# Turning the probabilities in 32x32 blocks on VectorE, and summing the values by matmuls of 32 rows, in the attention stage of a fused attention and expert kernel

## The chip, the cores and the metric

The kernel runs on one core of one Trainium2 chip. The time of a run is the device time of one execution in microseconds (us). Five engines work side by side and meet at semaphores: TensorE (PE; its weight loads are shown apart as PEld), VectorE (DVE), ScalarE (ACT), GpSimd (POOL) and SyncE (SP), which issues most DMAs.

## The reference

Three stages follow one another, and their only output is that of the last:

```python
scores = q @ k.T / sqrt(64) + bias[h]        # 4 batches x 8 heads, 576 positions, 64 dims
attn = exp(scores - max) / sum               # softmax over the 576 keys
x = attn @ v                                 # -> 2304 tokens of 512
x = one expert of 8 for each token (relu MLP of 1024, weighted by its gate)
out = gated FFN of width 1536 on the RMS-normed x
```

The bias of a head comes from a small MLP of 32 hidden units on log(1+|i-j|)/log(1+i). All inputs and outputs are float32. The change touches only `attn @ v`.

## The kernel before, in words

The attention stage works on pairs: 16 pairs of heads, one pair (two heads of one batch) after the other. `each_pair` (L417) writes out pairs 0, 1, 14 and 15 and runs pairs 2 to 13 in a loop of two pairs. A pair has five slots: in slots 0 to 3 (s in the code) 128 queries of head 0 and 128 of head 1, and in slot 4 (`MIX`) the last 64 queries of both heads as one tile. A tile of 128 queries of one head is a unit, so a pair has 9 units (`TPP`).

A unit goes through these steps:

- `scores` (L434, PE): four matmuls of 288 columns (eight in the mixed unit) into PSUM banks 0 to 3. q and k are split into a high and a low part in the type fp32r, and each operand is taken in one pass.
- `add_bias` (L605, DVE): one custom instruction that adds the bias, writes `a_sc` and takes the row's minimum (of the negated scores).
- `exps` (L668, ACT): the exponentials into `a_pr`, with the row sum beside them. `a_pr` holds two slots.
- `turn` (L538, PE): nine transposes of 128x128 a slot, three each into PSUM banks 4, 5 and 6. After them the keys lie on the partitions.
- `keep` (L680, ACT, banks 4 and 6) and `keep_middle` (L615, DVE, bank 5): copies from PSUM into `a_pt`, which holds all 576 x 576 turned probabilities of two heads, for two pairs.

Once a pair, in the next pair's slots:

- `values` (L549, PE): for 256 queries in slot 1 and 320 in slot 3, ten fp32 matmuls each: 128 rows of keys, 64 columns of weights (v), the two heads in the left and right half of the array. The trace shows each as two matmul records. They sum in PSUM bank 7.
- `keep_out` (L692, ACT): copies of the sums into `a_ot`.
- `turn_back` (L567, PE): five matmuls that turn 128 tokens back and also give the router's logits.
- `normal` (L630, DVE): the reciprocals of the sums and two multiplications into `a_xp`, which SP stores as tokens.

Nothing but the order in which each engine's function is written, and the semaphores, sets the order of the work. On every engine the work for the next unit stands in front of the work on this slot: in slot s PE first does `scores` of slot s+1. The semaphores named in the prediction: `a_b` counts units whose bias is added, `a_e` units whose exponentials are done, `a_x` halves of `normal`, `a_oe` copies of `keep_out`.

GpSimd splits q and k of a later pair (`split_k` L361, `split_q` L379) out of what SP has loaded (`load_qk` L314); SP's order in a pair is load_qk for the pair after next, the stores of the pair before in two parts, and between them v of the next pair (`load_v` L321). Each fourth pair SP also reloads the bias of two heads.

## Time and profile before

| | us |
|---|---|
| median of 3 runs | 1076.95 |
| lowest, highest | 1076.26, 1078.61 |
| the profiled execution's own time | 1076.09 |
| its span, first to last instruction | 1074.2 |
| TensorE's mean granted clock | 0.994 of 2.4 GHz |
| bias stage, until about | 60 us |
| first transposes of pair 0, last of pair 15 | 63.2 and 329.2 us |
| expert and FFN stages | from 339 us |

PE is busy for 97% of the span, DVE for 69%, ACT for 44%, POOL for 19%. PE's busy time counts a matmul from its start to its modelled end, and matmuls overlap, so it says that PE has work in hand and not how fast that goes. A record's mean duration is longer than the distance at which records follow one another; where the prediction speaks of the distance, it divides a stretch by its records.

### The profile page before, as it was taken

What the parts mean: (1) busy time and instruction counts of PE and PEld (TensorE: products, weight loads), DVE (VectorE), ACT (ScalarE), POOL (GpSimd) and SP (SyncE); (2) the same over time, 40 slices, a digit from 0 to 9 for tenths busy, and PEclk for the clock granted to TensorE, in tenths of its full rate; (3) what the DMA queues carried; (4) which work ended last, traced back from release to release, by engine and by line L of the source; (5) the groups of instructions that cost most, each with busy time, mean ns of one, the idle gap of its engine ahead of it and who ended that gap; (6) DMA issues with size and microseconds to landing.
All of it is one profiled execution on the core that took longest, in us unless ns stands there. A gap on an engine that the chain in (4) does not pass through costs nothing.

```text
span 1074.2 us, 23115 instructions
## 1 busy us (share of the span) xinstructions
PE 1045.0 (97%) x7161; PEld 937.6 (87%) x7162; DVE 740.3 (69%) x1252; ACT 476.7 (44%) x975; POOL 203.6 (19%) x197
## 2 busy tenths in 40 slices
PE   5989999999999899999999999999999999999997
PEld 1368888888887899999999999999999999999996
DVE  8975656656564747757464499887777777767765
ACT  7987777777772525645343343131211211121111
POOL 2036444535330411222121000001000100100101
PEclk9999999999999899999999999999999999999999
DMA  4983755656411844534322160002100100100000
GB/s 144 303 231 87 188 120 116 187 114 187 110 44 42 304 160 166 199 102 145 114 90 81 56 231 1 1 0 81 39 20 0 59 0 4 55 0 0 30 1 30
DMA packets 84455, 103.14 MB, mean 96 GB/s; under 512 B 46817, under 2 KB 58129, under 8 KB 84417
## 3 DMA queue, kind: packets, MB, share of 16 engines
q1 hardware_dynamic: 80384, 89.30, 28.3%
q0 software_dynamic: 4032, 13.37, 3.6%
q8 instruction: 19, 0.31, 0.1%
q14 instruction: 20, 0.16, 0.0%
HBM read 77.26 MB, written 25.40 MB: 96 GB/s over the span
## 4 chain that ended last, share of the span: by engine, by line
PE 89%; DVE 2%; issue 1%; POOL 1%; ACT 1%; DMA 0%; POOLq 0%; DVEq 0%; ACTq 0%
PE psum L1733 27%; PE psum L1741 13%; PE psum L1246 11%; PE psum L1255 10%; PE psum L563 8%; PE psum L446 8%; PE psum L546 7%; PE psum L576 2%; PE psum L1232 1%; DVE f_eg L1688 0%; PE psum L1294 0%; DMA e_xin<-x_tokens,e_col 0%; PE psum L876 0%; DVE r_inq L991 0%; POOL e_xin L1198 0%
## 5 line engine op out<-in xcount | busy, mean ns | idle before, releaser
L1688 DVE RECIPROCAL f_eg<-f_eg 128x384 f32<-128x384 f32 x72 | 183.4, 2547 | 0.0
L1656 ACT ACTIVATE f_eg<-psum 128x384 f32<-128x384 f32 x72 | 35.4, 492 | 312.0 <-PE psum L1733 312.0
L611 DVE CUSTOM_DVE_ANT_0 a_sc<-psum,a_bias 128x576 f32<-128x576 f32 x144 | 105.4, 756 | 65.6 <-PE psum L446 59.4
L1733 PE MATMUL psum<-f_x,f_ghi 128*128 (+1 forms) x576 | 147.5, 337 | 0.4 <-DVE f_x L1549 0.4
L1733 PE MATMUL psum<-f_x,f_vhi 128*128 (+1 forms) x576 | 146.1, 334 | 0.0
L674 ACT ACTIVATE a_pr<-a_sc,a_nmax 128x576 f32<-128x576 f32 x144 | 111.1, 772 | 26.5 <-DVE a_nmax L611 21.8
L1733 PEld LDWEIGHTS psum<-f_x,f_ghi 128*128 128x128 f32 x576 | 105.8, 188 | 6.6 <-DVE f_x L1549 0.6
L1625 POOL DMA_INDIRECT out<-f_ob,f_cols x18 | 18.2, 1009 | 464.9 <-ACT f_ob L1642 316.9
L1733 PEld LDWEIGHTS psum<-f_x,f_vhi 128*128 128x128 f32 x576 | 104.0, 188 | 0.0
L446 PE MATMUL psum<-a_khi,a_qs 128*128 128x288 f32 x320 | 96.4, 322 | 0.8 <-issue 0.3
L1733 PE MATMUL psum<-f_x,f_glo 128*128 (+1 forms) x288 | 97.1, 337 | 0.0
L1733 PE MATMUL psum<-f_x,f_vlo 128*128 (+1 forms) x288 | 96.2, 334 | 0.0
L546 PE MATMUL psum<-ident,a_pr 128*128 128x128 f32 x720 | 93.0, 273 | 0.7 <-ACT a_pt L690 0.5
L1347 ACT ACTIVATE e_hhi<-psum 128x288 fp32r<-128x288 f32 x72 | 29.7, 412 | 135.3 <-PE psum L1246 134.2
L446 PE MATMUL psum<-a_klo,a_qs 128*128 128x288 f32 x320 | 87.9, 295 | 0.0
L1684 DVE TENSOR_SCALAR f_eg<-f_eg 128x384 f32<-128x384 f32 x72 | 26.4, 367 | 88.6 <-ACT f_eg L1656 87.4
L1255 PE MATMUL psum<-e_hhi,e_w2hi 128*128 128x288 f32 x288 | 87.4, 303 | 0.0
L1246 PE MATMUL psum<-e_xhi,e_w1hi 128*128 128x288 f32 x288 | 87.3, 303 | 0.0
L563 PE MATMUL psum<-a_pt,a_v 128*64 128x256 f32 (+1 forms) x640 | 84.7, 411 | 1.3 <-DVE a_xp L643 0.8
L1741 PE MATMUL psum<-f_ohi,f_alo 128*128 128x512 f32 x216 | 85.4, 396 | 0.0
L1246 PE MATMUL psum<-e_xlo,e_w1hi 128*128 128x288 f32 x288 | 85.4, 297 | 0.0
L1741 PE MATMUL psum<-f_olo,f_ahi 128*128 128x512 f32 x216 | 85.3, 395 | 0.0
(245 smaller groups left out, 2354.4 us busy)
## 6 DMA issues: line engine op xcount, KB each, us to landing
e_raw<-ew SPq DMA_DIRECT2D x16, 1024.0 KB, 5.5
bias_ihj<-b_res SPq DMA_DIRECT2D x36, 288.0 KB, 2.7
a_qraw<-q SPq DMA_DIRECT2D x32, 288.0 KB, 5.1
a_kraw<-k SPq DMA_DIRECT2D x32, 288.0 KB, 5.7
a_bias<-bias_ihj SPq DMA_DIRECT2D x16, 576.0 KB, 7.0
xn_t<-e_yn SPq DMA_DIRECT2D x8, 576.0 KB, 3.1
a_v<-v SPq DMA_DIRECT2D x32, 128.0 KB, 2.4
x_tokens<-a_xp SPq DMA_DIRECT2D x64, 64.0 KB, 1.7
```

The source lines that it names most:

```text
L446: mm = e.matmul(s_ps[:, h, half, 0:HALF], qs[:, u, c:c + P], k[:, u, a * S + half * HALF:a * S + (half + 1) * HALF], start=(i == 0), stop= ...
L546: mm = e.transpose(t_ps[g][:, P * k:P * k + P], pr[:, w, c:c + P], ident[:, :])
L563: mm = e.matmul(o_ps[64 * h:64 * h + 64, 0:n], vv[:, u, k, 64 * h:64 * h + 64], pt[:, u, block, q:q + n], start=(k == 0), stop=(k == 4))
L611: e.tensor_tensor_reduce(sc[:, h, :].rearrange("p (a s) -> p a s", a=2), s_ps[:, h, :, 0:HALF], bias[:, 2 * s + h, :].rearrange("p (c s) - ...
L674: mm = e.activation(pr[:, w, S * h:S * h + S], sc[:, h, :], ACT.Exp, bias=nmax[:, h:h + 1], scale=-1.0, accum_out=sums[:, u, 2 * s + h:2 * ...
L1246: mm = e.matmul(bank[:, 0:BT], w[:, k, :], x[:, u, k, :], start=(k == 0 and n == 0), stop=(k == KD - 1 and n == 2))
L1255: mm = e.matmul(banks.y[:, k, 0:BT], w[:, k * P:(k + 1) * P], h[:, f % 3, :], start=(f == 0 and n == 0), stop=(f == KF - 1 and n == 2))
L1347: e.activation(self.hhi[:, f % 3, :], self.banks.h[f % 2][:, 0:BT], ACT.Relu).then_inc(self.s_hh, 1)
L1656: e.activation(self.eg[:, k % 2, :], self.g_ps[k % 2][:, 0:CHUNK], ACT.Exp, scale=-1.0).then_inc(self.s_e, 1)
L1688: e.reciprocal(x, x).then_inc(self.s_c, 1)
L1733: mm = e.matmul(acc[:, 0:CHUNK], a, b, start=(q == 0 and i == 0), stop=(q == KD - 1 and i == 2))
L1741: mm = e.matmul(self.o_ps[t], x, y, start=(f == 0 and i == 0), stop=(f == KFF - 1 and i == 2))
```

## The change

`turn` moves to DVE. One instruction (`transpose`, for each unit) turns 18 blocks of 32x32 within each group of 32 partitions, from `a_pr` in SBUF to `a_pt` in SBUF; there are 9 a pair. PE's 45 transposes a pair and the copies `keep` and `keep_middle` are gone, and so is the extra ACT instruction of the mixed slot. Since a block stays in its group of 32 partitions, group g of `a_pt` holds, for all 18 blocks of 32 keys, only the queries 32g to 32g+31 of each tile.

`values` therefore takes 32 rows at a time. For each of 18 blocks of keys, 4 groups and 2 heads there is one fp32 matmul of 32 rows, 64 columns of weights and 128 or 160 moving columns: 144 a pair, each summed over 18 blocks in the bank (4 to 7) of its group. They are dealt out over slots 1, 2 and 3, six blocks (48 matmuls) a visit. `keep_out`, `turn_back` and both halves of `normal` come once a pair, at slot 4. `turn_back` now writes to banks 4 and 5.

v must lie in all four groups of partitions, so `load_v` copies a pair's v four times (a host-side reordering makes each copy contiguous). v of pair 0 is loaded at the start of the attention stage and no longer during the bias stage.

On PE, around slot 1, where the sums of the pair before begin. a_pt is the turned probabilities, a_pr the probabilities, a_khi and a_klo the two parts of k; this is the order before:

```order
L563 MATMUL psum<-a_pt,a_v 64x256 [waits a_x]
L563 MATMUL psum<-a_pt,a_v 64x256 x9
L441 REGISTER_ALU
L446 MATMUL psum<-a_khi,a_qs 128x288 [waits a_b]
L446 MATMUL psum<-a_klo,a_qs 128x288
L446 MATMUL psum<-a_khi,a_qs 128x288
L446 MATMUL psum<-a_klo,a_qs 128x288
L542 REGISTER_ALU [waits a_e]
L546 MATMUL psum<-ident,a_pr 128x128 [waits a_t0]
L546 MATMUL psum<-ident,a_pr 128x128 x2
```

and this the beginning of the same place after the change, on PE:

```order
L438 MATMUL psum<-a_khi,a_qs 128x288
L438 MATMUL psum<-a_klo,a_qs 128x288
L534 ISA
L535 ISA [waits a_v1]
L538 ISA [waits a_t]
L547 MATMUL psum<-a_pt,a_v 64x160 [waits a_x]
L547 MATMUL psum<-a_pt,a_v 64x128
L547 MATMUL psum<-a_pt,a_v 64x160
L547 MATMUL psum<-a_pt,a_v 64x128 x2
```

The matmuls of 64x256 have become 48 of 64x160 and 64x128, between the same two groups of score matmuls, and the transposes behind them have left PE.

On DVE, from the bias of slot 4 (a_bias4) to the next pair's slot 0 (a_bias0), before the change:

```order
L611 ISA a_sc,a_nmax<-psum,a_bias 128x576 [waits a_bias4]
L611 ISA a_nmax 128x1
L635 ISA
L636 RECIPROCAL a_rinv<-a_sums 128x9 [waits a_e]
L637 RECIPROCAL a_rinv<-a_sums 128x1
L638 ISA
L640 REGISTER_ALU [waits a_r]
L641 ISA [waits a_bk]
L642 REGISTER_ALU [waits a_st01]
L643 TENSOR_TENSOR a_xp<-psum,a_rinv 128x288 [waits a_pa]
L618 ISA
L627 COPY a_pt<-psum 128x3x128 [waits a_o,a_t]
```

and after it, on DVE, from the second bias of the next pair's slot 0 to the end of the pair:

```order
L589 ISA a_sc,a_nmax<-psum,a_bias 128x576 [waits a_e,a_bias0]
L589 ISA a_nmax 128x1
L601 STREAM_TRANSPOSE a_pt<-a_pr 128x18x32 [waits a_e]
L609 ISA
L610 RECIPROCAL a_rinv<-a_sums 128x9 [waits a_e]
L611 RECIPROCAL a_rinv<-a_sums 128x1
L612 ISA
L614 REGISTER_ALU [waits a_r]
L615 ISA [waits a_bk]
L616 REGISTER_ALU [waits a_st01]
L617 TENSOR_TENSOR a_xp<-psum,a_rinv 128x288 [waits a_pa]
```

The copy has become a transpose, and the whole of `normal` stands behind the last transpose of the pair.

The diff, cut to the attention stage:

```diff
-    LOOPS = """b_mm b_ev b_st0 b_st1 b_st2 b_st3 a_st00 a_st01 a_st10 a_st11 a_s a_b a_e a_t a_t0 a_t1 a_t2 a_o a_oe a_bk a_r a_x a_pa
+    LOOPS = """b_mm b_ev b_st0 b_st1 b_st2 b_st3 a_st00 a_st01 a_st10 a_st11 a_s a_b a_e a_t a_o a_oe a_bk a_r a_x a_pa
...
-def front_stages(sem, arena, psum, qt, kt, v, ww, wg, biasd, xd, ident, rt, small):
+def front_stages(sem, arena, psum, qt, kt, vt, ww, wg, biasd, xd, ident, rt, small):
...
-    HALVES = ((0, 2 * P), (2 * P, S - 2 * P))
-    pt = arena.at("a_pt", [P, 2, TPP, S], arena.PT)
+    Q = 32
+    NG, NK = P // Q, S // Q
+    VISITS = {1: range(0, 6), 2: range(6, 12), 3: range(12, NK)}
+    pt = arena.at("a_pt", [P, 2, NK, 2 * P + Q], arena.PT)
...
-    vv = place("a_v", [P, 2, 5, P])
...
+    vv = arena.at("a_v", [P, 2, NK, P], arena.FRONT)
...
-    t_ps, o_ps = [psum[:, 4 + g, :] for g in range(3)], psum[:, 7, :]
-    back_ps = [s_ps[:, 1, 0, :], o_ps]
+    o_ps = psum[:, 4:8, :]
+    back_ps = [psum[:, 4, :], psum[:, 5, :]]
...
-    s_kept = [sem.loop(f"a_t{g}") for g in range(3)]
...
     def load_qk(e, pair, u, halves=(0, 1)):
...
-    def load_v(e, pair, u, parts=range(4)):
-        va, vb = (v[bass.ds(pair % B * H + pair // B * 2 + h, 1), :, :] for h in range(2))
-        cuts = ((vv[:, u, 0:4, 0:64], va[:, 0:BLK, :].rearrange("a (k p) d -> p (a k) d", p=P)),
-                (vv[:, u, 0:4, 64:P], vb[:, 64:S, :].rearrange("a (k p) d -> p (a k) d", p=P)),
-                (vv[0:64, u, 4, 0:64], va[:, BLK:S, :].rearrange("a p d -> p (a d)")),
-                (vv[64:P, u, 4, 64:P], vb[:, 0:64, :].rearrange("a p d -> p (a d)")))
-        for i in parts:
-            e.dma_start(*cuts[i]).then_inc(s_v[u], 16)
+    def load_v(e, pair, u):
+        for g in range(NG):
+            e.dma_start(vv[Q * g:Q * g + Q, u, :, :].rearrange("p k d -> p (k d)"),
+                        vt[bass.ds(pair, 1), :, :].rearrange("a p n -> p (a n)")).then_inc(s_v[u], 16)
...
     def load_bias(e, hp, s):
...
     def set_constants(e):
...
-            e.memset(vv[:, u, 4, :], 0.0)
...
-        if step in (12, 14, 16, 20):
-            if step == 12:
-                e.wait_ge(s_init, sem.at(s_init, 3))
-            load_v(e, 0, 0, ((12, 14, 16, 20).index(step),))
...
+            if h == 0:
+                e.wait_ge(s_init, sem.at(s_init, 3))
...
     def split_done(e, p):
...
-        if s == 0 and h == 1 and from_pair(p, 2):
-            e.wait_ge(s_x, sem.at(s_x, p * 2 - 3))
...
         def pair(p, u, uses):
...
+                load_v(e, 0, 0)
...
-                    e.wait_ge(s_o, sem.at(s_o, p * 2))
+                    e.wait_ge(s_o, sem.at(s_o, p))
...
     def tensor(e):
...
-        def turn(p, u, s, g):
-            n, w = p * SLOTS + s, (u + s) % 2
-            e.wait_ge(s_e, sem.at(s_e, p * TPP + min(2 * s + (2 if g else 1), TPP)))
-            e.wait_ge(s_kept[g], sem.at(s_kept[g], n))
-            for k in range(3):
-                block = 3 * g + k
-                c = P * block if s != MIX or block < 5 else 64 + P * (block - 5)
-                mm = e.transpose(t_ps[g][:, P * k:P * k + P], pr[:, w, c:c + P], ident[:, :])
-            mm.then_inc(s_t, 1)
-        def values(p, u, uses, half):
-            q, n = HALVES[half]
-            if half == 0:
-                e.wait_ge(s_v[u], sem.at(s_v[u], uses * 64 + 64))
-                for kept in s_kept:
-                    e.wait_ge(kept, sem.at(kept, p * SLOTS + SLOTS))
+        def values(p, u, uses, blocks):
+            if blocks[0] == 0:
+                e.wait_ge(s_v[u], sem.at(s_v[u], (uses + 1) * NG * 16))
+                e.wait_ge(s_t, sem.at(s_t, p * SLOTS + SLOTS))
+                sem.apart(e, p)
...
-            else:
-                e.wait_ge(s_oe, sem.at(s_oe, p * 2 + 1))
-            for k in range(5):
-                for h in range(2):
-                    block = 4 if k == 4 else 5 * h + k
-                    mm = e.matmul(o_ps[64 * h:64 * h + 64, 0:n], vv[:, u, k, 64 * h:64 * h + 64],
-                                  pt[:, u, block, q:q + n], start=(k == 0), stop=(k == 4))
-            mm.then_inc(s_o, 1)
-        def turn_back(p, half):
-            e.wait_ge(s_oe, sem.at(s_oe, p * 2 + half + 1))
-            if half == 0:
-                e.wait_ge(s_b, sem.at(s_b, min(p * TPP + 2 * TPP - 1, NPAIR * TPP) if isinstance(p, int) else p * TPP + 2 * TPP - 1))
-                if isinstance(p, int) and p == 0:
-                    e.wait_ge(s_wg, sem.at(s_wg, 32))
-            for t in range(2 + half):
-                c = P * (2 * half + t)
-                mm = e.matmul(back_ps[half][:, 2 * XW * t:2 * XW * (t + 1)], ot[:, c:c + P],
+                    sem.apart(e, p)
+            for k in blocks:
+                for g in range(NG):
+                    rows = slice(Q * g, Q * g + Q)
+                    for h in range(2):
+                        mixed = g // 2 == h
+                        first = 0 if h == 0 else P if mixed else P + Q
+                        n, to = P + Q * mixed, 0 if h and mixed else Q
+                        mm = e.matmul(o_ps[64 * h:64 * h + 64, g, to:to + n], vv[rows, u, k, 64 * h:64 * h + 64],
+                                      pt[rows, u, k, first:first + n], start=(k == 0), stop=(k == NK - 1))
+            if blocks[-1] == NK - 1:
+                mm.then_inc(s_o, 1)
+        def turn_back(p):
+            e.wait_ge(s_oe, sem.at(s_oe, p + 1))
+            if isinstance(p, int) and p == 0:
+                e.wait_ge(s_wg, sem.at(s_wg, 32))
+            for t in range(SLOTS):
+                half, at = t // 2 if t < MIX else 1, t % 2 if t < MIX else 2
+                mm = e.matmul(back_ps[half][:, 2 * XW * at:2 * XW * (at + 1)], ot[:, P * t:P * t + P],
...
-            mm.then_inc(s_bk, 1)
+                if t in (1, MIX):
+                    mm.then_inc(s_bk, 1)
...
         def pair(p, u, uses):
             for s in range(SLOTS):
...
-                if s in (1, 3) and from_pair(p, 1):
-                    values(p - 1, 1 - u, uses - 1 + u, s // 2)
-                if s == 3 and from_pair(p, 1):
-                    turn_back(p - 1, 0)
+                if s in VISITS and from_pair(p, 1):
+                    values(p - 1, 1 - u, uses - 1 + u, VISITS[s])
...
-                for g in range(3):
-                    turn(p, u, s, g)
...
-                    turn_back(p - 1, 1)
+                    turn_back(p - 1)
...
-        for half in range(2):
-            values(last, 1, NPAIR // 2 - 1, half)
-        for half in range(2):
-            turn_back(last, half)
+        values(last, 1, NPAIR // 2 - 1, range(NK))
+        turn_back(last)
...
     def vector(e):
...
-        def keep_middle(p, u, s):
-            n = p * SLOTS + s
-            e.wait_ge(s_t, sem.at(s_t, n * 3 + 2))
-            e.wait_ge(s_o, sem.at(s_o, p * 2 - 2))
-            t = t_ps[1]
-            if s == MIX:
-                e.tensor_copy(pt[:, u, 3, BLK:S], t[:, 0:64])
-                e.tensor_copy(pt[0:64, u, 4, BLK:S], t[0:64, P:P + 64])
-                e.tensor_copy(pt[64:P, u, 4, BLK:S], t[64:P, P + 64:2 * P])
-                e.tensor_copy(pt[:, u, 5, BLK:S], t[:, 2 * P + 64:3 * P]).then_inc(s_kept[1], 1)
-            else:
-                e.tensor_copy(pt[:, u, 3:6, s * P:s * P + P], t[:, 0:3 * P].rearrange("p (k q) -> p k q", k=3))\
-                    .then_inc(s_kept[1], 1)
+        def turn(p, u, s):
+            unit, n, w = p * TPP + 2 * s, p * SLOTS + s, (u + s) % 2
+            if s == 0:
+                e.wait_ge(s_o, sem.at(s_o, p - 1))
+            for h in range(1 if s == MIX else 2):
+                at = P if s == MIX else (P + Q) * h + Q * s
+                e.wait_ge(s_e, sem.at(s_e, unit + h + 1))
+                t = e.transpose(pt[:, u, :, at:at + Q], pr[:, w, S * h:S * h + S].rearrange("p (k q) -> p k q", q=Q))
+            t.then_inc(s_t, 1)
...
         def normal(p, u, uses, half):
...
-                if s == 3 and from_pair(p, 1):
-                    normal(p - 1, 1 - u, uses - 1 + u, 0)
...
-                keep_middle(p, u, s)
+                turn(p, u, s)
...
-                    normal(p - 1, 1 - u, uses - 1 + u, 1)
+                    for half in range(2):
+                        normal(p - 1, 1 - u, uses - 1 + u, half)
...
         def exps(p, u, uses, s, h):
...
-            e.wait_ge(s_t, sem.at(s_t, n * 3 - 3))
+            e.wait_ge(s_t, sem.at(s_t, n - 1))
...
-            if s == MIX:
-                mm = e.activation(pr[64:P, w, S:S + 64], sc[64:P, 0, 0:64], ACT.Exp, bias=nmax[64:P, 0:1], scale=-1.0)
...
-        def keep(p, u, s, g):
-            n = p * SLOTS + s
-            e.wait_ge(s_t, sem.at(s_t, n * 3 + g + 1))
-            e.wait_ge(s_o, sem.at(s_o, p * 2 - 2))
-            t = t_ps[g][:, 0:3 * P].rearrange("p (k q) -> p k q", k=3)
-            if s == MIX:
-                half = 32 * g
-                e.activation(pt[:, u, 3 * g:3 * g + 3, BLK:S], t[:, :, half:half + 64], ACT.Copy).then_inc(s_kept[g], 1)
-            else:
-                e.activation(pt[:, u, 3 * g:3 * g + 3, s * P:s * P + P], t, ACT.Copy).then_inc(s_kept[g], 1)
-        def keep_out(p, half):
-            q, n = HALVES[half]
-            e.wait_ge(s_o, sem.at(s_o, p * 2 + half + 1))
-            e.wait_ge(s_bk, sem.at(s_bk, p * 2 + half - 1))
-            mm = e.activation(ot[:, q:q + 2 * P], o_ps[:, 0:2 * P], ACT.Copy)
-            if half:
-                if isinstance(p, int) and p == 0:
-                    e.wait_ge(s_zero, sem.at(s_zero, 2))
-                for h in range(2):
-                    rows = slice(64 * h, 64 * h + 64)
-                    mm = e.activation(ot[rows, BLK + 64 * h:BLK + 64 * h + 64], o_ps[rows, 2 * P:n], ACT.Copy)
+        def keep_out(p):
+            e.wait_ge(s_o, sem.at(s_o, p + 1))
+            e.wait_ge(s_bk, sem.at(s_bk, p * 2))
+            e.activation(ot[:, 0:BLK].rearrange("p (t g q) -> p t g q", t=MIX, g=NG),
+                         o_ps[:, :, Q:Q + P].rearrange("p g (t q) -> p t g q", t=MIX), ACT.Copy)
+            if isinstance(p, int) and p == 0:
+                e.wait_ge(s_zero, sem.at(s_zero, 2))
+            for h in range(2):
+                rows, at, to = slice(64 * h, 64 * h + 64), 0 if h else Q + P, BLK + 64 * h
+                mm = e.activation(ot[rows, to:to + 64].rearrange("p (g q) -> p g q", g=2), o_ps[rows, 2 * h:2 * h + 2, at:at + Q], ACT.Copy)
...
         def pair(p, u, uses):
             for s in range(SLOTS):
...
-                if s in (2, 4) and from_pair(p, 1):
-                    keep_out(p - 1, s // 2 - 1)
+                if s == MIX and from_pair(p, 1):
+                    keep_out(p - 1)
...
-                keep(p, u, s, 0)
...
-                keep(p, u, s, 2)
...
-        for half in range(2):
-            keep_out(NPAIR - 1, half)
+        keep_out(NPAIR - 1)
...
     def exp_table(e):
...
+    vp = v.reshape(B, H // 2, 2, S // 32, 32, D).transpose(1, 0, 4, 3, 2, 5).reshape(NPAIR, 32, S * 2 * D // 32)
...
-        "q": np.ascontiguousarray(qp), "k": np.ascontiguousarray(kp.reshape(NPAIR, D, 2 * S)), "v": v.reshape(B * H, S, D),
+        "q": np.ascontiguousarray(qp), "k": np.ascontiguousarray(kp.reshape(NPAIR, D, 2 * S)), "v": np.ascontiguousarray(vp),
...
```

## Rows read from the trace of the kernel before

**Rows 1.** Busy time by stretch: one round of the loop, pair 0, pair 15, its tail.

```profile
core 0: us, PE busy (x) PEld busy (x) DVE busy (x) ACT busy (x) POOL busy (x), PEclk, DMA share, GB/s
126.68:160.91 34.23, 34.23 (x273) 28.43 (x272) 20.75 (x60) 24.98 (x67) 16.82 (x12) 1.00 0.58 130
63.20:75.62 12.42, 11.61 (x86) 10.16 (x86) 9.77 (x27) 11.51 (x31) 5.13 (x6) 1.00 0.63 169
314.87:329.30 14.43, 14.41 (x115) 11.23 (x112) 7.57 (x23) 10.27 (x27) 0.24 (x1) 1.00 0.08 19
329.30:338.60 9.30, 7.91 (x59) 5.15 (x58) 1.86 (x8) 1.65 (x7) 0.35 (x1) 1.00 0.10 24
```

**Rows 2.** Chain that ended last, within that round, by line.

```profile
by line: PE psum L446 33.1%; PE psum L563 30.1%; PE psum L546 28.8%; PE psum L576 8.3%
```

**Rows 3.** That round by line: busy us, mean ns, idle before.

```profile
L611 DVE CUSTOM_DVE_ANT_0 a_sc<-psum,a_bias 128x576 f32<-128x576 f32 x18 | 13.2, 756 | 8.4 <-PE psum L446 7.9 <-ACT a_pr L674 0.3
...
L546 PE MATMUL psum<-ident,a_pr 128*128 128x128 f32 x91 | 11.8, 273 | 0.0
...
L627 DVE COPY a_pt<-psum 128x384 f32<-128x384 f32 x8 | 4.4, 554 | 0.0
```

**Rows 4.** Timeline of PE around slot 1: start, us, instruction, records.

```profile
128.27 0.29 PE L446 MATMUL psum<-a_klo,a_qs 128*128 128x288 f32 x1
128.50 2.38 PE L563 MATMUL psum<-a_pt,a_v 128*64 128x256 f32 x20
130.80 0.40 PE L446 MATMUL psum<-a_khi,a_qs 128*128 128x288 f32 x1
```

**Rows 5.** Critical pieces of values: start, length, records.

```profile
128.56 2.31 PE psum L563 x20
135.69 2.84 PE psum L563 x20
```

**Rows 6.** Timeline of one step of the bias stage, PE.

```profile
40.73 1.18 PE L267 MATMUL psum<-b_hid,b_wc 128*32 128x288 f32 x16
```

**Rows 7.** Timeline of DVE: two bias units and a copy.

```profile
133.34 0.76 DVE L611 CUSTOM_DVE_ANT_0 a_sc<-psum,a_bias 128x576 f32<-128x576 f32 x1 [0.28 <-PE psum L446]
...
134.02 0.75 DVE L611 CUSTOM_DVE_ANT_0 a_sc<-psum,a_bias 128x576 f32<-128x576 f32 x1
...
134.70 0.55 DVE L627 COPY a_pt<-psum 128x384 f32<-128x384 f32 x1
```

**Rows 8.** Other DVE instructions of the whole run, by form.

```profile
L1688 DVE RECIPROCAL f_eg<-f_eg 128x384 f32<-128x384 f32 x72 | 183.4, 2547 | 0.0
...
L140 DVE TENSOR_SCALAR b_hid<-b_table,b_shift 128x576 f32 x96 | 41.3, 519 | 0.0
...
L643 DVE TENSOR_TENSOR a_xp<-psum,a_rinv 128x432 f32<-128x432 f32 x16 | 9.6, 600 | 1.2 <-PE psum L576 1.0
...
L643 DVE TENSOR_TENSOR a_xp<-psum,a_rinv 128x288 f32<-128x288 f32 x16 | 7.3, 458 | 44.4 <-PE psum L576 29.8 <-issue 14.6
...
L636 DVE RECIPROCAL a_rinv<-a_sums 128x9 f32<-128x9 f32 x16 | 3.3, 209 | 0.0
...
L357 DVE TENSOR_TENSOR a_klo<-a_kraw,a_khi 128x1152 fp32r<-128x1152 f32 x1 | 1.4, 1365 | 0.0
```

**Rows 9.** Timeline of POOL and SP: the split of q and k, its loads.

```profile
173.65 1.15 POOL L371 CAST a_khi<-a_kraw 128x1152 fp32r<-128x1152 f32 x1 [8.85 <-DMA a_kraw<-k]
...
181.86 0.35 POOL L510 TENSOR_TENSOR r_part<-r_part,a_xp 128x80 f32 x1 [0.31 <-POOL a_qs L391]
...
167.27 0.55 SPq L318 DMA_DIRECT2D a_kraw<-k  x1
```

**Rows 10.** DMA issues of the run: KB each, us from issue to landing.

```profile
e_raw<-ew SPq DMA_DIRECT2D x16, 1024.0 KB, 5.5
...
a_kraw<-k SPq DMA_DIRECT2D x32, 288.0 KB, 5.7
...
a_v<-v SPq DMA_DIRECT2D x32, 128.0 KB, 2.4
```


## The prediction

> **What bounds the kernel now.** I looked first at the stretches, to see which engine is full where. In a round of the attention loop (two pairs, 34.23 us) PE is busy without a gap, DVE for 20.75 us and ACT for 24.98 us, at the full granted clock [rows 1]. A busy PE says little by itself, so I read next the chain of waits within that round: it never leaves PE. Scores are 33.1% of it, values 30.1%, transposes 28.8%, turning back 8.3% [rows 2]. A pair takes 34.23 / 2 = 17.11 us, which makes 5.66 us of scores, 5.15 of values, 4.93 of transposes and 1.42 of turning back. DVE has 10.4 us of work a pair, and by lines its idle time is spent waiting for score matmuls (7.9 us a round) [rows 3]. So PE sets the pace, and DVE has 6.7 us of room in each pair.
>
> **What goes.** All 4.93 us of transposes leave the critical engine. The copies leave too, four of 0.55 us and some small ones on DVE, and ten on ACT, which isn't late anywhere and stays so.
>
> **What values costs in pieces of 32 rows.** Before, 20 records of 256 columns take 2.31 us of the chain and 20 of 320 take 2.84 [rows 5]. Both go as ten rounds of two records, the two heads side by side: the difference is 0.53 us for 640 columns, 0.83 ns a column, two cycles at 2.4 GHz, and 2.31 - 2560 x 0.00083 = 0.18 us is fixed. That columns of the array run side by side is plainest in the bias stage: 16 records of 288 columns on four groups of 32 columns end within 1.18 us [rows 6], while one after the other they'd need 16 x 288 x 0.83 ns = 3.8 us. They go as four rounds of four. The last record still in flight is part of the 1.18, so the rounds take about 0.24 us each, which is 288 columns.
>
> After the change a visit has 48 matmuls, 96 records, and eight tiles of the array (four groups of rows, two of columns) can take them: 12 rounds. A round lasts as long as its longest record, 160 x 0.83 = 0.133 us. A visit is 12 x 0.133 + 0.18 = 1.78 us, and 0.16 for the change from full-height to 32-row matmuls: the first record of values stands 0.23 us behind the last score matmul, where score matmuls follow each other at about 0.13 [rows 4]; I take a little more. V = 1.94 us. Three visits are 5.8 us a pair against 5.15, so no gain there: the sum of 576 keys costs as many cycles as before. What no row shows is that groups of rows run side by side as groups of columns do. From below V is bounded by the mean of 144 columns, 12 x 0.12 + 0.18 = 1.6; from above by one group of rows at a time, 48 x 0.133 + 0.34 = 6.7. I take 1.94, because the nearest row, the bias stage, gives full overlap of groups.
>
> The Trainium skill, "TensorE: Matmul & The Clock Gate", section "Measured speedup vs the span model", gives 3.07 times for four row tiles and 10.6 times for 16 row and column tiles. That would put the visit near my value; no run here shows it.
>
> **What a transpose costs on DVE.** No row shows one. The nearest of the same shape is the bias unit: 128x576, 0.76 us by itself, and the next one starts 0.68 us after it; a copy of 384 elements out of PSUM is 0.55 [rows 7]. A one-operand instruction on 576 elements in SBUF takes 0.43 (41.3 / 96), two operands of 1152 elements 1.37, a reciprocal 2.55 for 384 elements, which at 576 would be 3.8 [rows 8]. So T lies between 0.43 and 3.8 us. I take 0.75, one element a cycle like the bias unit, and a little more for reading whole blocks.
>
> **The new pace.** DVE's work a pair is 9 x 0.68 (bias) + 9 x 0.75 (transposes) + `normal`, 0.46 + 0.60 + 0.21 [rows 8] and a tiny reciprocal, 1.3: 14.2 us. PE's is 5.66 + 5.8 + 1.42 = 12.9. Neither is 17.1, but they don't overlap fully, since DVE takes its work in order. In slots 1 to 3 the second bias unit waits for the scores that PE has behind a visit, and this slot's transposes are queued behind that unit; ACT and PE wait for these in turn. So in these three slots PE sets the pace: 8 score records x 0.13 + V = 3.0 us, 9.0 in all. In slots 4 and 0 PE has only scores and turning back, and DVE sets it: 4 x 0.68 + 3 x 0.75 + 1.3 = 6.3. A pair then takes 15.2 us, or 3V + 3T + 7.2. The floor is DVE's own 9T + 7.4.
>
> At the pair's end there is a new chain: `keep_out`, `turn_back` and `normal` now come once, and values of the next pair wait for `a_x`, since both use banks 4 and 5. The wait is passed because one slot of scores and transposes (3 us) lies between; if it isn't, it costs up to 1 us a pair, which the range holds.
>
> **The sum.** Pairs 1 to 14: 14 x (17.11 - 15.2) = 26.7 us. Pair 15 took 14.43 [rows 1]; it has 7 bias units, 9 transposes and one `normal` on DVE, 4.8 + 6.8 + 1.3 = 12.9: 1.5 saved. Pair 0 has no values; 12.42 becomes 9 x 0.68 + 9 x 0.75 = 12.9, 0.5 lost. The tail of 9.3 us keeps its size: 36 rounds are 4.8 us against 5.15. In all -27.7, against the profiled execution's own 1076.09: 1048.4. The median of the runs is 0.9 above that execution, so I say 1049.
>
> **DMA.** Four copies of v are 1.15 MB a pair where 0.29 were. A load of 1 MB lands 5.5 us after its issue [rows 10]. SP issues v ahead of the next q and k, and now only at the pair's end, since the first store waits for `normal`. Before, k was issued at 167.27, and GpSimd split it from 173.65 to 181.9 [rows 9]; the pair had begun at 160.91 [rows 1], and its scores come in slot 4 of the next pair, near 191.5. The cover is 9.6 us. The change eats 2.4 of issue and up to 6 of transfer, and two shorter pairs 3.8; if v takes all of that, the cover is gone. Transfers share their engines with q and k rather than go strictly ahead, so I count nothing but keep it as a case. v of pair 0, 2.3 MB with that of pair 1, has pair 0's 13 us to land.
>
> **Rivals.**
>
> *Transposes are slow.* VectorE turns four-byte blocks at half rate, T = 1.36 as for 1152 elements [rows 8]. DVE becomes the bound: 9 x 1.36 + 7.4 = 19.6 us a pair, 15 x 2.5 = 38 us more, 1114. It decides from T = 1.08. For it: nothing shows the operation. Against: every DVE row of one pass in this kernel but the reciprocal is at one element a cycle or better.
>
> *Row groups do not overlap as I think.* If only half of the eight tiles run at a time, V = 24 x 0.133 + 0.34 = 3.5, and PE is the bound with 3V + 7.1 + some 1.5 of hand-over = 19.1: 1106. If one group at a time, V = 6.7, 28.7 us a pair: 1250. It decides from V of about 2.8. For it: eight tiles need the engine to look 32 instructions ahead, four needed 16 (two loads and two matmuls a tile). Against: the full overlap of four tiles [rows 6].
>
> *A fixed price per record.* Records in this trace are never sustained closer than 0.06 us (0.24 / 4) [rows 6], and V needs 1.6 / 96 = 0.017. Were the 0.06 a limit of issue and not the columns' own time, V = 5.9 and the time 1215; but it is exactly 288 columns' time, so I count it with the case above. The Trainium skill, "TensorEngine Tiling (Array Packing)", section "Instruction Overhead", speaks against the change: each matmul costs about 60 cycles, 25 ns, however few its columns. As an estimate from that page V would be 2.4 + 0.34 = 2.7 and the pair 17 us: no gain, 1077. No row here shows it. By rows alone, the case is that a record costs 0.025, between the 0.017 needed and the 0.06 seen; its time is 1077.
>
> *k comes late.* If the DMAs take all of what I allowed, the pair settles where the cover is zero: 9.6 - 8.4 = 1.2 = 2 x (17.11 - P), P = 16.5, time 1067.
>
> **Chances.** Forecast as laid out (1038 to 1060): 0.55. Late k (1067): 0.10. Fixed price per record (1070 to 1080): 0.08. Half of the tiles (1106): 0.07. One group at a time or worse (1200 and up): 0.08. Slow transposes (1114): 0.12. A difference under 0.2%, 2 us, can't be told from none. Faster: 0.55 + 0.10 + a part of the 0.08, 0.66; same 0.04; slower 0.30. The range leaves out the case above 1200 and holds the rest: 1036 to 1116; the forecast's own range is 1038 to 1060.
>
> **What the profile after would show.** The DVE transposes' mean, 0.7 to 0.85; the values' 96 records within about 2 us a visit, records starting a few ns apart; the distance of a pair 15.2; DVE the fullest engine of the loop, over 90% busy; the critical chain changing between values and DVE's bias units and transposes; ACT under 60%; the granted clock still at 1.0 of 2.4 GHz. I'd be wrong if a visit took over 2.8 us, if a transpose took over 1.08, or if GpSimd's split of k ended after PE asks for it.

## The result, and the profile after

The changed kernel takes 1093.32 us (median of 4 runs, 1092.23 to 1095.44), the kernel before 1076.89 beside it: 1.0152 times as long, 95% interval 1.0132 to 1.0172. It is 16 us slower where 28 us were to be gained, 44 us over the forecast. The profiled execution spans 1092.1 us.

I measure a pair from its first bias unit to the next pair's; the marks of [rows 1] lie 2.7 us later in a pair. Stretches of the changed kernel, the columns as in [rows 1]: pairs 5 and 6, pair 7 with a reload of the bias, pair 8, and pairs 1 and 2.

```profile
158.76:173.84 15.08, 13.45 (x339) 11.56 (x338) 13.49 (x32) 8.54 (x22) 7.90 (x5) 1.00 0.69 155
173.84:189.25 15.41, 13.48 (x339) 11.56 (x338) 13.61 (x32) 8.56 (x22) 7.88 (x5) 1.00 0.78 173
189.25:210.48 21.23, 14.99 (x349) 12.84 (x348) 13.47 (x32) 9.05 (x24) 8.77 (x6) 0.94 0.86 210
210.48:227.34 16.86, 14.64 (x328) 12.59 (x328) 13.57 (x32) 7.98 (x19) 7.01 (x5) 0.77 0.91 226
75.20:98.70 23.50, 15.72 (x330) 13.40 (x330) 12.64 (x28) 8.70 (x21) 8.61 (x5) 0.72 0.73 155
98.70:120.50 21.80, 17.53 (x342) 15.19 (x341) 13.80 (x32) 8.11 (x20) 9.73 (x6) 0.84 0.56 124
```

An undisturbed pair takes 15.1 to 15.4 us, where [rows 1] gave 17.11 and the forecast said 15.2. The others are the loss. Against 15.2 us each, pairs 1 and 2 (23.5 and 21.8) lose 14.9 us; 3, 7 and 11, which reload the bias (21.3, 21.2, 19.9), lose 16.8; the pairs behind these (17.1, 16.9, 17.4) lose 5.7; the other six together 1.5, all of it in pair 14 (16.7). Pair 0 adds 0.7, pair 15 with the tail, up to the start of the last write of `a_xp`, 4.4 (29.9 us; 27.0 before, less the 1.5 of the forecast). The sum is 44.

Two forms by line, as in [rows 3], over the attention stage, then one visit (as [rows 4]) and the two transposes beside it:

```profile
L589 DVE CUSTOM_DVE_ANT_0 a_sc<-psum,a_bias 128x576 f32<-128x576 f32 x144 | 104.8, 743 | 65.3 <-PE psum L438 47.6 <-DMA a_bias<-bias_ihj 15.7 <-issue 1.0
L601 DVE STREAM_TRANSPOSE a_pt<-a_pr 128x576 f32<-128x576 f32 x144 | 103.9, 756 | 0.0
```

```profile
170.39 1.43 DVE L601 STREAM_TRANSPOSE a_pt<-a_pr 128x576 f32<-128x576 f32 x2
...
170.70 1.91 PE L547 MATMUL psum<-a_pt,a_v 32*64 32x160 f32 x96
```

The visit and the transpose cost what the forecast gave them. What the forecast didn't have is the DMA wait in the first row, new in this size. Here it is on DVE, at the end of pair 7:

```profile
202.87 1.43 DVE L601 STREAM_TRANSPOSE a_pt<-a_pr 128x576 f32<-128x576 f32 x2
210.45 0.76 DVE L589 CUSTOM_DVE_ANT_0 a_sc<-psum,a_bias 128x576 f32<-128x576 f32 x1 [6.15 <-DMA a_bias<-bias_ihj]
```

And this is what stood ahead of the bias in SyncE's queue.

```profile
192.74 1.04 SPq L452 DMA_DIRECT2D x_tokens<-a_xp  x2
194.15 1.75 SPq L324 DMA_DIRECT2D a_v<-v  x4
196.29 1.08 SPq L459 DMA_DIRECT2D x_tokens<-a_xp  x2
197.61 1.33 SPq L462 DMA_DIRECT2D x_tokens<-a_xp  x2
199.30 0.54 SPq L317 DMA_DIRECT2D a_qraw<-q  x1
...
202.45 2.43 SPq L334 DMA_DIRECT2D a_bias<-bias_ihj  x4
```

The pair began at 189.25. The stores wait for `normal`, which DVE now runs behind the last transpose of pair 6, from 191.3 to 192.75; v is behind them, q and k behind v, and the bias, 2.6 MB, behind all, 13.2 us into a pair that lasts 15. In the kernel before, whose pair 7 began at 175.40, v was issued 0.9 us into the pair and the bias 9.7:

```profile
176.27 2.36 SPq L328 DMA_DIRECT2D a_v<-v  x4
...
183.95 0.55 SPq L318 DMA_DIRECT2D a_kraw<-k  x1
185.14 2.38 SPq L337 DMA_DIRECT2D a_bias<-bias_ihj  x4
```

### The profile page after: what moved, and what is told of

Read it like the earlier page. It is cut to its first block, busy times and chain, and to the rows that moved or that the text cites. A ratio compares the mean times of both kernels' runs of the same rounds, so it can differ in the third digit from the quotient of the medians.

```text
span 1092.1 us, 28659 instructions
## 1 busy us (share of the span) xinstructions
PE 1006.4 (92%) x10409; PEld 913.6 (84%) x10410; DVE 790.5 (72%) x1268; ACT 413.6 (38%) x783; POOL 202.6 (19%) x195
## 4 chain that ended last, share of the span: by engine, by line
PE 65%; DVE 2%; issue 1%; ACT 1%; POOL 1%; DMA 0%; POOLq 0%; DVEq 0%; ACTq 0%
PE psum L1688 27%; PE psum L1696 13%; PE psum L1201 11%; PE psum L1210 10%; PE psum L1187 1%; PE psum L547 1%; DVE f_eg L1643 0%; PE psum L1249 0%; DMA e_xin<-x_tokens,e_col 0%; PE psum L559 0%; PE psum L831 0%; PE psum L849 0%; PE psum L438 0%; POOL e_xin L1153 0%; POOL e_col L1149 0%
## 5 line engine op out<-in xcount | busy, mean ns | idle before, releaser
L438 PE MATMUL psum<-a_khi,a_qs 128*128 128x288 f32 x320 | 104.4, 345 | 34.7 <-DVE a_nmax L589 30.4
L438 PEld LDWEIGHTS psum<-a_khi,a_qs 128*128 128x128 f32 x320 | 65.1, 204 | 56.8 <-DVE a_nmax L589 40.8
L547 PE MATMUL psum<-a_pt,a_v 32*64 32x128 f32 (+1 forms) x4608 | 102.0, 312 | 9.6 <-issue 8.8
L547 PEld LDWEIGHTS psum<-a_pt,a_v 32*64 32x64 f32 x4608 | 86.3, 140 | 21.2 <-issue 21.2
L601 DVE STREAM_TRANSPOSE a_pt<-a_pr 128x576 f32<-128x576 f32 x144 | 103.9, 756 | 0.0
L438 PE MATMUL psum<-a_klo,a_qs 128*128 128x288 f32 x320 | 94.1, 312 | 3.7 <-issue 3.7
```

The costliest lines, as they stand in the source:

```text
L438: mm = e.matmul(s_ps[:, h, half, 0:HALF], qs[:, u, c:c + P], k[:, u, a * S + half * HALF:a * S + (half + 1) * HALF], start=(i == 0), stop= ...
L547: mm = e.matmul(o_ps[64 * h:64 * h + 64, g, to:to + n], vv[rows, u, k, 64 * h:64 * h + 64], pt[rows, u, k, first:first + n], start=(k == 0 ...
L601: t = e.transpose(pt[:, u, :, at:at + Q], pr[:, w, S * h:S * h + S].rearrange("p (k q) -> p k q", q=Q))
```

## The experiments

The kernel before, run beside each, took 1076.6 to 1077.5 us. Line numbers shift by a few between kernels.

**Is it the bias?** The first run leaves the reload out, so that later heads get the bias of the first two.

```diff
-            if not isinstance(p, int) and u == 1:
-                with e.If(uses % 2 == 1):
-                    for s in range(SLOTS):
...
-            e.wait_ge(s_bias[s], sem.at(s_bias[s], (p // B + 1) * (32 if s == MIX else 16)))
+            e.wait_ge(s_bias[s], 32 if s == MIX else 16)
```

> The changed kernel without the reload of the bias in pairs 3, 7 and 11: all pairs add the bias of the first two heads (this part of the computation is left out). Theory A, the bias comes late: in the changed kernel VectorE waits 15.7 us in all for a_bias at the ends of these three pairs, the half granted clock follows, and the next pair takes 16.9 to 17.4 us where others take 15.1. Without the reload pairs 3, 7, 11 fall from 21.3, 21.2 and 19.9 us to 15.1 to 15.4, the pairs behind them from 17.1, 16.9 and 17.4 to 15.1 to 15.4, no low clock behind them: 1093 - 17.4 - 5.8 = 1070, at least 1075. Rival B, the four copies of v slow the transfers of k, q and stores throughout, and the reload only happens to stand there: at most 3 us are gained and another wait (for a_kraw or the split) takes its place. The first pairs (13.6, 23.5, 21.8 us) stay as they are in both.

1071.96 us, ratio 0.9946 (0.9928 to 0.9963): 21.4 us less. Pairs 5 to 13 take 14.95 to 15.24 each, and the granted clock stays at 1.00 through them. Pair 3 still takes 17.9, and pairs 1 and 2 stay at 23.9 and 21.6. Theory A holds. The counterpart on the kernel before:

> The kernel before without the reload of the bias in pairs 3, 7 and 11 (this part of the computation is left out), the counterpart of the first run on the changed kernel, where this gave 21.4 us. Theory A, the reload was hidden but for 1.9 us of waits: 1074 to 1077. Rival G, each reload costs both kernels the same, by contention: 1060 or less.

1074.85 us, ratio 0.9982 (0.9973 to 0.9992), 2.1 us. So the same reload costs at most 2 us there and 21 here. In the two traces the attention stage from pair 1 on is only 0.8 us shorter: VectorE waited 0.7 us for a reload, and the rest of the 1.9 us that the expectation names was in pair 0, where nothing is reloaded.

**Its place in the queue, or the bytes?** First the reload on ScalarE's queue, with v, q and k left as they were:

```diff
...
+                if not isinstance(p, int) and u == 1 and s in (1, 3):
+                    with e.If(uses % 2 == 1):
+                        for t in ((0, 1, 2) if s == 1 else (3, MIX)):
+                            load_bias(e, (p // B + 1) % (H // 2), t)
```

> The changed kernel with the reload of the bias issued from ScalarE's queue as soon as the bias units of a slot are done (three slots in slot 1, two in slot 3 of pairs 3, 7, 11), where SyncE issues it behind the stores, v, q and k. Theory A1, what makes the bias late is its place in SyncE's order (issued 13.9 us after the first bias unit of the pair where it was 9.7): it lands before the pair's end, and pairs 3, 7, 11 take 15.1 to 16 us: 1070 to 1076. Theory A2, the transfers themselves are too slow since v's four copies share the DMA engines: the landing only moves by the issue and over half of the 15.7 us of waiting stays: 1083 or more. ScalarE has 40% of idle time in a pair; five issues of its queue cost it well under 3 us in each of these pairs.

1087.85 us (1082.88 to 1090.06), ratio 1.0094 (1.0058 to 1.013). The time is theory A2's, but not by the wait that it named: pair 7 fell to 15.1, as A1 said, and pair 8 rose to 19.8:

```profile
211.77 1.15 POOL L367 CAST a_khi<-a_kraw 128x1152 fp32r<-128x1152 f32 x1 [13.34 <-DMA a_kraw<-k]
...
220.09 0.39 PE L438 MATMUL psum<-a_khi,a_qs 128*128 128x288 f32 x1 [1.92 <-POOL a_qs L387]
```

k, issued until 198.40 behind v and the stores, with the bias on the same DMA engines, is there 13 us later, and TensorE waits for its split. That is the rival "k comes late" of the prediction, brought on by the cure. The wait moved from one transfer to the next. Then fewer bytes, each issue in its place:

```diff
+        n = NK if isinstance(pair, int) and pair < 2 else 5
-            e.dma_start(vv[Q * g:Q * g + Q, u, :, :].rearrange("p k d -> p (k d)"),
-                        vt[bass.ds(pair, 1), :, :].rearrange("a p n -> p (a n)")).then_inc(s_v[u], 16)
+            e.dma_start(vv[Q * g:Q * g + Q, u, 0:n, :].rearrange("p k d -> p (k d)"),
+                        vt[bass.ds(pair, 1), :, 0:n * P].rearrange("a p n -> p (a n)")).then_inc(s_v[u], 16)
```

> The changed kernel with fewer bytes of v and the same order: from pair 2 on each of the four loads brings 5 of 18 key blocks, 80 KB where 288 KB were, so that a pair loads 0.32 MB of v, as before the change (the rest of v is stale: this part of the computation is left out). Same number of issues, at the same places. Theory A, in pairs 3, 7 and 11 bias (2.6 MB), v, q and k ask for more than the DMAs bring in the pair's time: with 0.8 MB less, 3.3 us at the 250 GB/s of that stretch, the wait for a_bias falls from 4.7-5.5 us to about 2 in each, the pairs behind it keep a part of the half clock: 1080 to 1086. Rival E, the place in SyncE's order alone: bias is issued 13.9 us into the pair whatever v moves, the waits stay within 1 us: 1090 to 1093.

The time, 1058.09 us, can't be used as it stands: this kernel leaves most of v stale, and the expert stage is 27 us shorter, probably because tokens then go to other experts (249.6 from the last a_xp to the first matmul of the stage behind it, 276.9 in the changed kernel). The attention stage is comparable: 286.8 us from the first bias unit to the last a_xp, 295.2 in the changed kernel. The 8.4 us are what pair 2 (16.4) and pair 15 with the tail (26.8) give; the gains and losses of the other pairs cancel. Pairs 3, 7 and 11 take 23.3, 19.3 and 19.5, and VectorE waits 16.6 us for a_bias in them (15.7 in the changed kernel). Rival E holds for the reload. The last check on bytes puts them into the kernel before:

```diff
+    def load_more(e, pair, u):
+        for g in range(3):
+            e.dma_start(more_v[32 * g:32 * g + 32, u, :],
+                        kt[bass.ds(pair, 1), :, :].rearrange("a (p b) s -> p (a b s)", b=2)).then_inc(s_v[u], 16)
...
```

`load_more` stands behind each `load_v`, for pair 0 at the start of the attention stage, and `values` waits for it too.

> The kernel before with three more loads of 288 KB a pair behind those of v, from k into a place that nothing reads, so that its DMAs carry as much as the changed kernel's (1.15 MB a pair instead of 0.29). Theory A, the bytes alone do little harm at 17.1 us a pair: waits for a_bias grow from 1.9 us to some 3 to 8 in all, 1078 to 1085. Rival B, the four copies slow q and k throughout: every pair grows, 1090 or more.

1088.61 us, ratio 1.0108 (1.0088 to 1.0129), 3.6 us above what theory A expected at most, and not where rival B had it. Pairs 1 to 3 take 23.1, 19.5 and 19.2 (16.5, 17.4, 17.0 before), pairs 7 and 11 17.8 and 17.9, and the others up to 13 17.0 to 17.2. The bytes hurt most at the start, where q and k of pair 2 stand behind v of pair 1 and the added loads of two pairs:

```profile
POOL a_khi L377 <- DMA a_kraw<-k: 27.8, 2, 19.5
...
PE psum L452 <- POOL a_qs L397: 5.8, 1, 5.8
```

**The start.** q and k of pair 2 ahead of v:

```diff
-            if isinstance(p, int) and p == 0:
-                load_v(e, 0, 0)
-                load_v(e, 1, 1)
             if not (isinstance(p, int) and p >= NPAIR - 2):
                 split_done(e, p)
                 load_qk(e, p + 2, u)
+            if isinstance(p, int) and p < 2:
+                load_v(e, p, u)
```

> The changed kernel with SyncE's order at the start changed: q and k of pair 2 go ahead of v of pair 0, and v of pair 1 behind q and k of pair 3; before, both v (8 loads of 288 KB) went first. Theory A, k of pair 2 comes late behind 2.3 MB of v (GpSimd waits 21 us for a_kraw until 89.4, its split ends at 97.3, TensorE waits for it): pairs 1 and 2 fall from 23.5 and 21.8 us to 15.5 to 18 each: 1078 to 1082. Rival C, these pairs are long because each engine runs code for the first time (fetch gaps of 3.7 and 3.5 us on TensorE) and at half the granted clock: they fall by less than 4 us together, 1089 to 1093. Pairs 3, 7, 11 stay as they are in both.

1091.95 us, ratio 1.0138 (1.0121 to 1.0155), the time of rival C, but with its cause not shown by it. GpSimd's wait for k went, but v of pair 0 is late instead, and pair 1 stays at 24.0 us; pair 2 gains 2.4.

```profile
84.57 1.90 PE L546 MATMUL psum<-a_pt,a_v 32*64 32x160 f32 x50 [4.25 <-DMA a_v<-v]
```

**SyncE's order as a whole.** If one queue holds everything behind the stores' wait, the cure is to issue what is free first:

```diff
-                load_qk(e, p + 2, u)
...
+            if reload:
+                with e.If(uses % 2 == 1):
+                    bias_again(p, range(3))
+            if reload:
+                with e.If(uses < NPAIR // 2 - 2):
+                    qk_ahead(p, u)
+            elif not isinstance(p, int) or p + 3 < NPAIR:
+                qk_ahead(p, u)
...
+            if reload:
+                with e.If(uses % 2 == 1):
+                    bias_again(p, range(3, SLOTS))
             if from_pair(p, 1):
-                store_first(p - 1, 1 - u)
                 if not (isinstance(p, int) and p == NPAIR - 1):
                     e.wait_ge(s_o, sem.at(s_o, p))
                     sem.apart(e, p)
                     load_v(e, p + 1, 1 - u)
+                store_first(p - 1, 1 - u)
                 store_second(p - 1, 1 - u)
```

Here `qk_ahead` is `split_done(e, p + 1)` and the load of q and k of pair p + 3, and `bias_again` the reload of the slots named, with their waits. At the start, q and k of pairs 2 and 3 now stand between v of pair 0 and v of pair 1.

> The changed kernel with another order on SyncE alone. In each pair: the bias of slots 0 to 2 (where it is reloaded), then q and k of three pairs ahead as soon as GpSimd has split the pair whose buffer they take, then the bias of slots 3 and 4, then v as soon as the values that used its buffer are summed, and the stores, which wait for `normal` at the pair's end, last. At the start v of pair 0, q and k of pairs 2 and 3, v of pair 1. In the changed kernel q, k, v and the bias all stand behind the stores' wait. Theory A, nothing but this order makes the bias and k late: pairs 3, 7, 11 take 15.1 to 16.5 us (were 21.3, 21.2, 19.9), the pairs behind them 15.1 to 15.5, pair 1 and 2 stay long in part: 1093 - 16 - 5 - 3 = 1069, between 1062 and 1074, faster than before the change. Rival F, the DMA engines are full there whatever the order (the second run with the bias issued early by ScalarE only moved the wait to k in the pair behind): at most half of it comes back, 1080 to 1088.

1063.82 us (1062.19 to 1066.68), ratio 0.988 (0.9857 to 0.9902): 29.5 us less than the changed kernel and 13 less than the kernel before. Pair 7 and its bias:

```profile
179.20:194.30 15.10, 13.46 (x339) 11.56 (x338) 13.49 (x32) 8.54 (x22) 7.91 (x6) 1.00 0.84 229
```

```profile
187.51 1.76 SPq L334 DMA_DIRECT2D a_bias<-bias_ihj  x3
...
192.92 0.34 SPq L334 DMA_DIRECT2D a_bias<-bias_ihj  x1
```

The bias is issued 8.3 us into the pair. The DMAs move 229 GB/s at a share of 0.84, where they moved 210 at 0.86 in the bad pair of the changed kernel: rival F, engines that are full whatever the order, falls. Pairs 5 to 14 take 151.9 us in all, 15.2 each. Pair 14 is back at 14.8, and the tail gives back 3.1 of its 4.4 us. Which part of the order does it? Only q and k moved ahead, the diff above without the bias and v:

> The changed kernel with only q and k issued ahead as in the run with SyncE's new order (three pairs ahead, as soon as their buffer is split; at the start q and k of pairs 2 and 3 between v of pair 0 and of pair 1); v stays behind the first stores, and the bias behind v, q and k. Theory A, in pairs 3, 7, 11 it is the bias that comes late, and k only behind it: it is issued at about the same time as in the changed kernel (14 us into the pair, since q and k wait for the split), waits of 4 to 6 us for a_bias stay, those pairs take 19 to 21 us; the start gains as in the new order (pair 1 18.3 us, pair 2 22.4): 1080 to 1088. Rival J, k was the loss: pairs 3, 7, 11 fall to 15.1 to 16.5 and the time to 1062 to 1068.

1086.91 us, ratio 1.0094 (1.0077 to 1.0111). Pairs 1 and 2 (18.9 and 20.6) give 5.8 of the 6.4 us; pairs 3, 7 and 11 still take 22.2, 19.9 and 19.8:

```profile
DVE a_sc L602 <- DMA a_bias<-bias_ihj: 14.3, 3, 4.8
```

The other 23.1 us belong to the bias and v ahead of the stores, which no run separates. And the same order on the kernel before:

> The kernel before with SyncE's new order (q and k three pairs ahead, the bias of slots 0 to 2 ahead of them, v as soon as its buffer is free, the stores last). Theory A, nothing there waited for SyncE but 1.9 us for a_bias: 1075 to 1077. Rival K, the new order is worth as much to the kernel before as to the changed one (29 us): 1050 or less, and then the change itself is no gain.

1076.98 us, ratio 1.0 (0.999 to 1.0009). The order is worth nothing there; the 13 us are the change's own, once its queue is in order.

**Eight tiles or fewer.** Two runs turn the loops of a visit, with the same 96 records. Groups outermost, so that two tiles take turns:

```diff
-            for k in blocks:
-                for g in range(NG):
+            for g in range(NG):
+                for k in blocks:
```

> The changed kernel with the loop over the four row groups outside the loop over the six key blocks of a visit, so that six rounds of two tiles follow each other in one group of rows before the next group comes; the same 96 records, sums and banks. In the changed kernel a visit takes 1.91 us. Theory A, the eight tiles run side by side because consecutive records name different tiles, within some 32 instructions of look-ahead: with the loops turned, records of one group (24 records, up to 6 deep on a tile) queue on two tiles: a visit lies between 1.9 (the look-ahead reaches over groups) and 4 x 6 x 0.133 + 0.34 = 3.5 us (only two tiles at a time); I expect 3 to 3.5, TensorE becomes the bound with 3 x 3.3 + 7.1 + 1.5 = 18.5 us a pair, and the time is 1125 to 1145. Rival D, TensorE runs tiles side by side whatever their order: 1.9 us and the time unchanged. If so, the price per record and not the columns sets 1.91 us (96 x 0.020).

1383.46 us (1377.03 to 1425.1), ratio 1.282 (1.2771 to 1.2869). Then, on the kernel with the new order, two groups at a time:

```diff
-            for k in blocks:
-                for g in range(NG):
+            for k, g in [(k, 2 * half + g) for half in range(2) for k in blocks for g in range(2)]:
```

> The kernel with SyncE's new order (1063.8 us), the records of a visit in another order: first all key blocks for row groups 0 and 1, then all for groups 2 and 3, so that four tiles take turns where eight did and two did in the run with the groups outside (5.30 us a visit at the full granted clock, 0.110 us for each of 48 steps of two records). Theory A, what consecutive records name decides, a step of all tiles in turn costs 0.11 to 0.13 us: 24 steps, 2.7 to 3.3 us a visit. TensorE then needs 3 x 3.0 + 7.1 = 16.1 us a pair and some hand-over, 16.5 to 18.5 us: 14 pairs x 2.3 = 32 us more, 1085 to 1112. Rival D, the price is per record once at least four tiles take turns: 1.9 to 2.2 us a visit and 1064 to 1070.

1162.05 us (1154.99 to 1180.1), ratio 1.0794 (1.0766 to 1.0822). A visit at the full granted clock, two tiles and four:

```profile
482.33 5.30 PE L547 MATMUL psum<-a_pt,a_v 32*64 32x160 f32 x96
```

```profile
232.70 3.02 PE L562 MATMUL psum<-a_pt,a_v 32*64 32x160 f32 x96
```

5.30 us for 48 steps, 3.02 for 24, 1.91 for 12. What consecutive records name decides; rival D falls in both. The columns still set the pace of a tile: in the changed kernel's visit records of 160 columns follow each other on their tile at 0.136 us, those of 128 at 0.109, which is 0.85 ns a column. With two tiles in turn a step is 0.110, since the next group's records begin as soon as the tile with 128 columns has taken its last. But both runs are longer than their visits, by another cause. Two pairs of the second, one at each granted clock:

```profile
227.40:245.80 18.40, 16.49 (x339) 14.86 (x338) 13.57 (x31) 8.51 (x21) 7.90 (x6) 1.00 0.94 212
245.80:273.90 28.10, 26.47 (x338) 23.90 (x338) 13.48 (x31) 8.52 (x21) 10.94 (x8) 0.61 0.45 99
```

A pair of 16.5 to 18.5 was expected, and most are. Every third pair takes 28 instead, one of these at a mean granted clock of 0.61 with TensorE busy 94% of it, 90% in the pair before it; what sets it off is open.

**The pace.** The values in four visits, to test the sum of slots:

```diff
-    VISITS = {1: range(0, 6), 2: range(6, 12), 3: range(12, NK)}
+    VISITS = {0: range(0, 3), 1: range(3, 8), 2: range(8, 13), 3: range(13, NK)}
```

> The kernel with SyncE's new order (1063.8 us), the values of a pair in four visits instead of three: 3 key blocks in slot 0 and 5 in each of slots 1 to 3, where it was 6 in each of slots 1 to 3. It tests the pace that the forecast's sum is made of: slots 1 to 3 at TensorE's pace, slots 4 and 0 at VectorE's. Visits measured so far: 5.30 us in 48 steps of two tiles, 3.02 in 24 of four, 1.91 in 12 of eight; a visit of 5 blocks has 10 steps: at 0.133 us each and 0.34 fixed 1.7 us, one of 3 blocks 1.1 to 1.3. Slots 1 to 3 take 3 x (1.04 + 1.7) = 8.2 us instead of 9.0, slots 4 and 0 stay at 6.3 since TensorE has room there: 14.5 us a pair. Theory L, the sum of slots holds: pairs of 14.4 to 14.7 us, 1063.8 - 14 x 0.6 = 1055, between 1052 and 1059. Rival M, the first visit comes before the last transposes and `normal` of the pair before are done and TensorE waits in slot 0: pairs of 15.1 us or more, 1063 to 1075.

1072.79 us, ratio 0.9963 (0.995 to 0.9976): 9 us slower than with three visits; rival M. Pairs 3 to 13 take 15.95 to 16.17, but for pair 12 with 19.3: in this trace, which is 4 us above the median, it waits 2.0 us for the bias reloaded in pair 11, and its granted clock is 0.91. The visits have the size given, but the first waits for `normal`:

```profile
185.02 1.07 PE L563 MATMUL psum<-a_pt,a_v 32*64 32x160 f32 x48 [0.86 <-DVE a_xp L633]
187.27 1.64 PE L563 MATMUL psum<-a_pt,a_v 32*64 32x160 f32 x80
```

**First-time code.** With the new order pairs 1 to 4 still take 18.3, 22.4, 16.7 and 16.0 us. The changed kernel has gaps there that nothing releases, as within this visit:

```profile
107.81 0.75 PE L547 MATMUL psum<-a_pt,a_v 32*64 32x160 f32 x19
112.06 2.66 PE L547 MATMUL psum<-a_pt,a_v 32*64 32x128 f32 x77 [3.50 <-issue]
```

So the loop, which runs its body six times, was written out for four pairs:

```diff
-        with e.Fori(0, NPAIR // 2 - 2) as it:
-            pair(it * 2 + 2, 0, it + 1)
-            pair(it * 2 + 3, 1, it + 1)
+        with e.Fori(0, NPAIR // 4 - 1) as it:
+            for j in range(2):
+                pair(it * 4 + 2 * j + 2, 0, it * 2 + j + 1)
+                pair(it * 4 + 2 * j + 3, 1, it * 2 + j + 1)
```

> The kernel of the run with SyncE's new order (1063.8 us), with the attention loop written out for four pairs instead of two, run three times instead of six; the same instructions in the same order on every engine. Question: the first pairs are still long there (18.3, 22.4, 16.7, 16.0 us where 15.1 is the pace), with gaps of 3.6 and 4.4 us on TensorE that nothing in the trace releases, each near a fetch of instructions. Theory H, code that runs for the first time costs: pairs 4 and 5, which were the loop's second pass, now run code for the first time: each grows by 0.5 to 3 us over 15.1 to 15.4, fetches appear between 149 and 185 us, and the time is 1065 to 1070. Rival I, the first pairs are long because transfers and the clock need time to settle: pairs 4 and 5 stay at 15.1 to 15.4 and the time within 1 us of 1063.8.

1104.77 us (1100.26 to 1107.09), ratio 1.0269 (1.025 to 1.0288): 41 us from code that says the same. That is over six times what theory H expected, because fetching goes on in all three passes: from 150 to 290 us there are 24 fetches of 16 KB on the instruction queue, and none in the kernel with a loop of two pairs. How the 41 us divide between the stalls and the lower clock beside them (0.92 from 148 to 345 us) isn't taken apart. The first row is the queue's (packets, MB, share), the others are visits that it breaks:

```profile
q8 instruction: 24, 0.39, 1.3%
```

```profile
216.50 0.97 PE L564 MATMUL psum<-a_pt,a_v 32*64 32x160 f32 x27 [2.54 <-issue]
219.63 2.23 PE L564 MATMUL psum<-a_pt,a_v 32*64 32x160 f32 x92
223.69 0.49 PE L564 MATMUL psum<-a_pt,a_v 32*64 32x128 f32 x4 [1.83 <-issue]
```

The counterpart on the kernel before, six pairs written out and run twice:

> The kernel before with its attention loop written out for six pairs and run twice. TensorE's queue has 616 instructions in a round of two pairs there (18 a us), 1392 in the changed kernel's (46 a us, 100 a us within a visit); six pairs are 1850, so that six pairs more run code for the first time, and perhaps all twelve do. The same writing out, for four pairs, cost the changed kernel 41 us. Theory N, it is the rate that hurts: a fetch brings 16 KB, 256 instructions, and in the changed kernel's loop of four they follow each other at 3.5 to 4.1 us, 62 to 73 instructions a us, which 18 a us never ask for: 1076 to 1080, with 1 to 2 us for jumps. Rival O, any code that isn't at hand costs stalls of 2 to 5 us at each fetch: 7 or more fetches, 1095 and up.

1085.42 us, ratio 1.0074 (1.0057 to 1.0091), between the two. It fetches 12 times in the same 140 us, yet all its pairs but one take what they took, 16.5 to 17.4. The one, 26.6 us, holds the loop's jump back:

```profile
203.08 0.60 PE L447 MATMUL psum<-a_khi,a_qs 128*128 128x288 f32 x1 [7.05 <-issue]
```

TensorE has 18 instructions a us there and 46 in the changed kernel, 100 within a visit. Fetches in sequence didn't hurt at the first rate and came with stalls at the second, as theory N says; that the rate is the cause is argued, since the two kernels differ in more. A jump back to code that is gone stopped TensorE for 3.9 and 5.2 us in the loop of four pairs and for 7.0 here, which N had at 1 to 2.

## Why the prediction was wrong

**Right.** V, 1.91 us against 1.94, with columns at 0.85 ns for 0.83, and 12 steps of it: visits of 12, 10 and 6 steps take 1.91, 1.64 and 1.07, so 0.14 a step where I had 0.133. T, 0.756 against 0.75. The pace of 15.2 us, in part by luck (see the sum of slots). ScalarE 56% busy. DVE is 89% busy, not over 90, and TensorE has 13.4 us a pair where I summed 12.9. The rivals on transposes, row groups and price per record fall: a record costs 1.91 / 96 = 0.020 us. The Trainium skill, "TensorEngine Tiling (Array Packing)", section "Instruction Overhead", has about 60 cycles a matmul, 25 ns at 2.4 GHz. This trace shows less a record, and on different tiles the first eight records of a visit start 7 ns apart; the trace decides. The Trainium skill, "TensorE: Matmul & The Clock Gate", section "Measured speedup vs the span model", has 3.07 times for four row tiles; four row groups (with two column tiles in both) against one are 5.30 / 1.91 = 2.8 here.

**The step that failed: "so I count nothing".** The forecast put the DMA term at nothing. I wrote that SyncE issues v "only at the pair's end, since the first store waits for `normal`", and followed only q and k behind it. The reload of the bias stands in the same queue, behind these, in three pairs of sixteen; I had looked at rounds without one. It had been hidden but for 2 us at most. Moving the stores' wait to the pair's end pushed it from 9.7 us into the pair to 13.2, in a pair 2 us shorter. Leaving it out gives 21.4 us; with q and k already ahead, moving the bias and v ahead of the stores gives 23.1. The loss of these pairs is more than the 15.7 us of waiting, since the granted clock falls behind each wait (0.77 in pair 8) and the pair after it takes 17 us.

**v of pair 0 "has pair 0's 13 us to land".** So it has, but q and k of pair 2 were behind it. Moving them is worth 6.4 us, and putting the same bytes into the kernel before costs it 11.6. k late was a rival, placed in the steady pairs; there it stays hidden. At the start my own sign of being wrong came true: TensorE waits 4.1 us for GpSimd's split.

**A term that was missing.** With the queue in order the time is 14.8 us over the forecast; 12.5 of it lie in pairs 1 to 4 (73.3 us against 60.8). These run new code with 2.3 times as many instructions as before, at half the granted clock in part. The written-out loops show that fetching can cost such sums, and in these pairs TensorE stands for 8.6 us in three gaps that nothing releases (3.3, 4.1 and 1.2 us). How the 12.5 divide between fetch, clock and transfers isn't settled, since no run took one away alone.

**The sum of slots** gave the right pace for three visits, and a wrong one for four (14.5 said, 16.0 measured). The right one is partly luck. Slots 1 to 3 were to go at TensorE's pace, 3.0 us each; in a steady pair the visits start 3.1 and 3.9 us apart, and VectorE waits little for scores, 1.3 of 15.1 us:

```profile
DVE a_sc L589 <- PE psum L438: 1.3, 2, 0.9
```

So VectorE, busy for 13.5 of the 15.1 us, sets most of the pair, TensorE's slots little of it. I had noted the wait for `a_x` as passed because a slot lies between. Take that slot away and it shows, with 0.9 us of the 1.5.

## What to carry to other kernels

When a wait moves later in a queue that issues DMAs in order, list everything behind it for every iteration, the rare ones too, and compare each issue with its deadline at the new, shorter pace. A transfer that is cured alone hands its wait to the next one, so the order of the queue is the thing to change. Where a change splits the same work into many short instructions, count instructions per us and the size of the loop's body, not only their columns.

## What the hardware showed that I had not expected

- Tiles run side by side by the order of the records alone: 96 records in 5.30, 3.02 or 1.91 us.
- TensorE's granted clock fell to half for 23.9 us at a time, once in three pairs, in a loop where it was 90 to 94% busy with four tiles, and not in the steady pairs with eight.
- A loop body of 1392 TensorE instructions isn't fetched again (no fetch from 150 to 290 us), one of about twice that is, in every pass (24 fetches). A jump back to a body that is gone stopped TensorE for 3.9 to 7.0 us.
- Transposes of 128x576 four-byte elements in 32x32 blocks take 0.756 us on VectorE, as long as a bias unit of that shape.
